# Attention's output stored unnormalised and scaled ahead of the first expert layer, row maxima placed by ScalarE

## The chip, the core and the metric

The kernel runs on one core of a Trainium2 chip. The metric is the device time of one execution in microseconds, as the median of several runs. TensorE (PE) multiplies matrices, VectorE (DVE), ScalarE (ACT) and GpSimd (POOL) work on tiles in SBUF, the first two on PSUM also, and SyncE's queue (SP) issues all DMAs here. The engines run their own instruction lists in order and wait for one another through semaphores.

## What is computed

Attention with rotary positions over 4 batches of 8 heads, 576 positions, 64 columns; its result, brought to 2304 tokens of 512 columns, goes through two expert layers without bias. All is in 32-bit floats.

```python
q_rot, k_rot = rotate(q), rotate(k)
scores = (1 / sqrt(64)) * q_rot @ k_rot.T
attn = exp(scores - max(scores, axis=-1))
attn = attn / (sum(attn, axis=-1) + 1e-9)
x = (attn @ v), heads side by side          # [2304, 512]
h = x @ w_in1;  x = (h - tanh(h)) @ w_out1   # 512 -> 2048 -> 512
h = x @ w_in2;  x = (h * sigmoid(1.702 h)) @ w_out2
```

## The kernel before, in words

**Attention.** 32 heads in 16 pairs. A product of 32-bit accuracy is made of parts: each operand is cut into an upper part (a copy by ScalarE into the format fp32r, `keys_hi` L551, `queries_hi` L557) and a lower part (the rest, a subtraction by VectorE, `keys_lo` L679, `queries_lo` L684). VectorE also rotates keys and queries (`rope`, L659 to L662).

In step h of the loop TensorE computes the transposed scores of head h in five tiles of 128 keys (`scores`, L431 and L437), and with a lag of two tiles the product of the exponentials with v (`probs_v`, L449). Between them it makes scores in the other orientation for the heads ahead (`near_scores`, L414): tiles 1 to 4 of head h+1 in the first two places, tile 0 of head h+2 at the end of the step. VectorE takes the row maxima of these (`row_max`, L667), TensorE transposes the five columns of maxima in the place t = 2 (`maxima_across`, L421), and `place_maxima` (L674, VectorE) multiplies the transposed rows with a 0/1 mask into five rows of `q_max`, where row t holds only the maxima of queries in tile t. The L437 matmuls against the rows of ones in `k_one` then subtract the maxima inside the scores' sum. The slots for scores, near scores and the transpose are three pairs of PSUM banks used in rotation, in the order of `ring_order` (L46 to L60): an operation waits until the third before it in that order has been read.

ScalarE's step h is: exp of each of the five tiles (L537), the copy of the previous head's output `copy_pv` (L545) at t = 1, the cut of x (L580) at t = 2 in the steps 17 and 19, the cut of weights (L573) at t = 3 in the steps 21, 23, 25, 27 and 31, then `keys_hi` at t = 3 and `queries_hi` at t = 4 for head h+3. VectorE's step h is: row maxima 1 to 4 of head h+1, one rope, `place_maxima`, the early cuts, `keys_lo` and `queries_lo` of head h+3, row maximum 0 of head h+2, and in even steps `invert` (L688).

**From attention to x.** v carries 64 columns of ones, so rows of `pv_sb` hold the sums. SP fetches a row of sums per head (`fetch_sums`, L231), VectorE adds 1e-9 and inverts, SP stores the inverses (`store_inverse`, L236), reads them back spread over 64 partitions twice (`spread_inverse`, L244), GpSimd multiplies (`normalise`, L382), and SP stores the pair (`store_x`, L249). `copy_pv` of a head waits until the buffer of four heads before has been multiplied.

**Expert layers.** 2304 tokens in 6 units of 384, 16 steps j per unit. `first_product` (L485) makes h for a step in 12 matmuls, ScalarE the tanh or sigmoid (L608, L610), VectorE g (L742), ScalarE its upper part (L617), VectorE its lower part (L747), `second_product` (L500, L503) another 12 or 9 matmuls, one step behind. At step 8 ScalarE and VectorE cut x for the next unit (L580, L703). In unit 0 they also cut the weights, five steps ahead (L573, L697). x of layer one is read in 768 KB pieces from DRAM by `load_x` (L261), half a unit or more ahead.

Of the kernel before, what the change touches and what calls it, by code (L numbers as in the profile page):

```python
# [6 lines left out]
F32 = mybir.dt.float32  # L7
# [58 lines left out]
def program(nc, q, k, v, w_in1, w_out1, w_in2, w_out2, cos_t, sin_t, out):  # L66
# [3 lines left out]
    inv_scratch = nc.dram_tensor("inv_scratch", [PAIRS, 2, SEQ], F32, kind="Internal").ap()  # L70
# [3 lines left out]
    with ExitStack() as ctx:  # L74
# [41 lines left out]
        inv_wide = [sb(f"inv_wide{j}", [P, SEQ], stack=one_stack) for j in range(2)]  # L116
        x_out = [sb(f"x_out{j}", [P, SEQ], stack=one_stack) for j in range(2)]
# [33 lines left out]
        inv_out = sem("inv_out")  # L151
        inv_in = [sem(f"inv_in{j}") for j in range(2)]
        norm_done = sem("norm_done")
        x_stored = [sem(f"x_stored{j}") for j in range(2)]
# [43 lines left out]
        def _(sp):  # L198
# [26 lines left out]
            def fetch_sums(h):  # L225
# [3 lines left out]
                if pair >= 2:  # L229
                    sp.wait_ge(inv_out, 16 * (pair - 1))  # L230
# [3 lines left out]
            def store_inverse(pair):  # L234
                sp.wait_ge(inv_done, pair + 1)
                sp.dma_start(inv_scratch[pair].rearrange("a (p j) -> (a p) j", j=SEQ // HD), sums[pair % 2][:, :]).then_inc(inv_out, 16)  # L236

            def spread_inverse(pair):
                par = pair % 2
                sp.wait_ge(inv_out, 16 * (pair + 1))  # L240
                if pair >= 2:
                    sp.wait_ge(norm_done, pair - 1)
                for a in range(2):
                    sp.dma_start(inv_wide[par][own(a), :], inv_scratch[pair, a:a + 1, :].broadcast_to([HD, SEQ])).then_inc(inv_in[par], 16)  # L244

            def store_x(pair):
                row, col = pair % PAIRS_PER_BATCH * P, pair // PAIRS_PER_BATCH * SEQ
                sp.wait_ge(norm_done, pair + 1)
                sp.dma_start(x_scratch[0][row:row + P, col:col + SEQ], x_out[pair % 2][:, :]).then_inc(x_stored[pair % 2], 16)  # L249

            def load_x(m, u):
# [3 lines left out]
                if m:  # L255
                    sp.wait_ge(y_stored, 16 * (u + 1))
                else:
                    batches = ((u + 1) * UNIT - 1) // SEQ + 1
                    for j in range(2):
# [24 lines left out]
            for h in range(-1, NHEADS):  # L284
# [27 lines left out]
            store_x(PAIRS - 2)  # L312
# [14 lines left out]
            spread_inverse(PAIRS - 1)  # L327
            for m in range(LAYERS):
                for u in range(UNITS):
# [25 lines left out]
        def _(pool):  # L355
# [5 lines left out]
            nc.gpsimd.memset(tile_mask, 0.0).then_inc(pool_chain, 1)  # L361
            pool.wait_ge(pool_chain, 2)
            nc.gpsimd.affine_select(out=tile_mask, in_=tile_mask, compare_op=ALU.not_equal, fill=1.0,
# [450 lines left out]
```

## Time and profile before

| | us |
|---|---|
| median of 3 runs | 1148.81 (1148.41 to 1148.97) |
| the profiled execution | 1147.27 |
| its span, first to last instruction | 1145.5 |
| mean granted TensorE clock | 0.997 |

Times in a profile count from the start of the span. A line of the timeline gives start, length in us, engine, code line, operation, output<-input and shapes; in square brackets how long the engine stood idle just before, and what released it. "x4" is four instructions told in one line. PEld is TensorE loading weights, which runs beside its matmuls. PEclk is the granted clock, 1.00 for full speed.

### The profile page before, as it was taken

Reading aid. Unit: us, or ns where it says so; the run is one execution under the profiler, and the core shown is the slowest. Engines: PE = TensorE matmul, PEld = TensorE weight load, DVE = VectorE, ACT = ScalarE, POOL = GpSimd, SP = SyncE. Lnnn points to the kernel's source line nnn. Section 1 sums busy time; section 2 is a strip of 40 time slices with the busy share of each in tenths; the row PEclk is TensorE's granted clock in tenths of the full one; section 3 lists DMA queues with packets and bytes.
Section 4 is the critical chain, followed back from the end, with each engine's and each line's share of the span. In section 5 each row is a group of like instructions: output and inputs, shape, how many; then the busy total and the mean of one; then the engine's idle time right before and its main releaser. Section 6 shows DMA issues by size and latency. Waiting matters only on the chain.

```text
span 1145.5 us, 15078 instructions
## 1 busy us (share of the span) xinstructions
PE 1104.1 (96%) x5952; PEld 1017.8 (89%) x5952; DVE 552.4 (48%) x879; ACT 425.7 (37%) x747; POOL 57.1 (5%) x62
## 2 busy tenths in 40 slices
PE   2999998999999999999999999999999999999998
PEld 1888877787789999999999999999999999999997
DVE  7888887888736433232233333455232322323222
ACT  2555554555544423222222323445232222323222
POOL 3011111102111000000000000000000000000000
PEclk9999999999999999999999999999999999999999
DMA  6355557566315300000000100062000000000000
GB/s 182 95 158 127 155 154 201 136 169 166 87 61 178 102 28 29 28 28 11 19 28 28 29 28 28 1 193 83 28 28 28 28 1 28 28 28 1 28 1 28
DMA packets 78854, 79.85 MB, mean 70 GB/s; under 512 B 30144, under 2 KB 55744, under 8 KB 78784
## 3 DMA queue, kind: packets, MB, share of 16 engines
q1 hardware_dynamic: 78784, 78.89, 24.1%
q8 instruction: 47, 0.77, 0.3%
q14 instruction: 23, 0.19, 0.1%
HBM read 55.12 MB, written 14.23 MB: 61 GB/s over the span
## 4 chain that ended last, share of the span: by engine, by line
PE 89%; DVE 7%; SPq 1%; DMA 1%; POOL 1%; issue 1%; ACT 0%; POOLq 0%; DVEq 0%; ACTq 0%
PE PS L485 35%; PE PS L503 17%; PE PS L500 17%; PE PS L449 10%; PE PS L414 3%; PE PS L431 3%; PE PS L437 3%; DVE neg_max L667 2%; DVE q_max L684 1%; DVE k_hl L679 1%; DVE q_max L674 1%; DMA turned_k<-k_dram 1%; DVE raw_q L662 0%; DVE w_parts L697 0%; DVE raw_q L660 0%
## 5 line engine op out<-in xcount | busy, mean ns | idle before, releaser
L485 PE MATMUL PS<-x_hi,w_parts 128*128 128x384 f32 x1536 | 423.1, 336 | 0.0
L742 DVE TENSOR_TENSOR g_raw<-PS,act_t 128x384 f32<-128x384 f32 x192 | 107.0, 557 | 400.2 <-ACT act_t L610 202.1
L485 PEld LDWEIGHTS PS<-x_hi,w_parts 128*128 128x128 f32 x1536 | 280.5, 188 | 4.3
L485 PE MATMUL PS<-x_lo,w_parts 128*128 128x384 f32 x768 | 257.2, 335 | 0.0
L500 PE MATMUL PS<-g_hi,w_parts 128*128 128x384 f32 x768 | 210.3, 334 | 0.8 <-DVE g_lo L747 0.8
L503 PE MATMUL PS<-w_parts,g_hi 128*128 128x512 f32 x576 | 195.1, 393 | 1.0 <-DVE y_sb L756 0.8
L449 PE MATMUL PS<-probs,v_one 128*128 128x288 f32 x640 | 183.4, 409 | 0.3 <-ACT pv_sb L545 0.3
L747 DVE TENSOR_TENSOR g_lo<-g_raw,g_hi 128x384 fp32r<-128x384 f32 x192 | 107.7, 561 | 113.6 <-ACT g_hi L617 113.6
L537 ACT ACTIVATE probs<-PS 128x576 f32<-128x576 f32 x160 | 104.0, 650 | 129.6 <-PE PS L437 126.3
L485 PEld LDWEIGHTS PS<-x_lo,w_parts 128*128 128x128 f32 x768 | 144.2, 188 | 4.2
L617 ACT ACTIVATE g_hi<-g_raw 128x384 fp32r<-128x384 f32 x192 | 100.8, 525 | 122.9 <-DVE g_raw L742 119.7
L500 PEld LDWEIGHTS PS<-g_hi,w_parts 128*128 128x128 f32 x768 | 140.0, 188 | 1.1 <-DVE g_lo L747 1.1
L449 PEld LDWEIGHTS PS<-probs,v_one 128*128 128x128 f32 x640 | 112.4, 191 | 18.1 <-issue 0.5
L667 DVE TENSOR_REDUCE neg_max<-PS 128x1 f32<-128x576 f32 x160 | 113.8, 746 | 30.1 <-PE PS L414 29.5
L500 PE MATMUL PS<-g_lo,w_parts 128*128 128x384 f32 x384 | 128.3, 334 | 0.0
L503 PEld LDWEIGHTS PS<-w_parts,g_hi 128*128 128x128 f32 x576 | 108.1, 188 | 21.9 <-issue 1.1
L610 ACT ACTIVATE act_t<-PS 128x384 f32<-128x384 f32 x96 | 47.2, 492 | 212.5 <-PE PS L485 212.5
L608 ACT ACTIVATE act_t<-PS 128x384 f32<-128x384 f32 x96 | 47.2, 492 | 206.9 <-PE PS L485 206.9
L414 PE MATMUL PS<-k_hl,q_hh 128*128 128x288 f32 x320 | 86.7, 376 | 34.8 <-DMA q_hh<-q_hh 17.5
L503 PE MATMUL PS<-w_parts,g_lo 128*128 128x512 f32 x288 | 113.7, 395 | 0.0
L414 PEld LDWEIGHTS PS<-k_hl,q_hh 128*128 128x128 f32 x320 | 56.4, 200 | 51.8 <-issue 19.7
L431 PE MATMUL PS<-q_hh,k_hl 128*128 128x288 f32 x320 | 80.0, 332 | 0.0
(51 smaller groups left out, 741.3 us busy)
## 6 DMA issues: line engine op xcount, KB each, us to landing
x_raw<-x_scratch SPq DMA_DIRECT2D x12, 768.0 KB, 4.5
raw_w<-moe_w_in_dram SPq DMA_DIRECT2D x32, 256.0 KB, 3.1
raw_w<-moe_w_out_dram SPq DMA_DIRECT2D x32, 256.0 KB, 3.3
raw_k<-k_dram SPq DMA_DIRECT2D x16, 288.0 KB, 3.5
turned_k<-k_dram SPq DMA_DIRECT2D x64, 72.0 KB, 3.2
raw_q<-q_dram SPq DMA_DIRECT2D x16, 288.0 KB, 3.8
turned_q<-q_dram SPq DMA_DIRECT2D x64, 72.0 KB, 3.5
k_one<-k_hl SPq DMA_DIRECT2D x32, 144.0 KB, 2.4
```

The lines of the kernel that those rows point to most:

```text
L414: last = nc.tensor.matmul(slot[:, b, :], q_hh[h % 4][:, t * P:(t + 1) * P], k_hl[h % 4][:, b * HALF:(b + 1) * HALF], start=True, stop=True)
L431: nc.tensor.matmul(slot[:, b, :], k_hl[h % 4][:, keys], q_hh[h % 4][:, b * HALF:(b + 1) * HALF], start=True, stop=False)
L449: last = nc.tensor.matmul(pv_banks[:, b, :], v_one[h // 2 % 2][:, h % 2, t, :], probs[g % PROBS][:, b * HALF:(b + 1) * HALF], start=t == 0 ...
L485: last = nc.tensor.matmul(h_banks[j % 2], w_parts[j][:, w, c * P:(c + 1) * P], x[par][:, c, :], start=(c == 0 and w == 0 and x is x_hi), s ...
L500: last = nc.tensor.matmul(acc_banks[c][:, 0:UNIT], w_parts[j][:, w, c * P:(c + 1) * P], g[:, s, :], start=start, stop=stop)
L503: last = nc.tensor.matmul(acc_banks[c], g[:, s, c * P:(c + 1) * P], w_parts[j][:, w, :], start=start, stop=stop)
L537: nc.scalar.activation(probs[g % PROBS][:, :].rearrange("p (b n) -> p b n", b=2), slot_halves(slot_of("S", h, t)), ACT.Exp).then_inc(exp_d ...
L608: nc.scalar.activation(act_t[:, j % 2, :], h_banks[j % 2], ACT.Tanh).then_inc(act_done, 1)
L617: nc.scalar.activation(g_hi[:, j % STAGES, :], g_raw[:, j % 2, :], ACT.Copy).then_inc(g_hi_done, 1)
L667: nc.vector.tensor_reduce(neg_max[h % 2][:, t:t + 1], slot_halves(slot_of("M", h, t)), AX.XY, ALU.max, negate=True).then_inc(max_done, 1)
L742: nc.vector.tensor_tensor(g_raw[:, j % 2, :], h_banks[j % 2], act_t[:, j % 2, :], ALU.subtract if m == 0 else ALU.mult).then_inc(g_done, 1)
L747: nc.vector.tensor_tensor(g_lo[:, j % STAGES, :], g_raw[:, j % 2, :], g_hi[:, j % STAGES, :].bitcast(F32), ALU.subtract).then_inc(g_lo_don ...
```

## The change

The multiplication by the inverse sums moves. `copy_pv`'s result is stored as it is, per head (`store_x(h)`), GpSimd's `normalise` and SP's `spread_inverse` are gone. The inverses are kept in DRAM by chunk and token; with each `load_x` of the first layer SP loads the inverses spread over 2 x 64 partitions into a new buffer `inverses`, and VectorE multiplies x in place (`scale_x`), early for unit 0 and at step 8 for the others. ScalarE's cut of x waits for it, and its early cut moves from t = 2 to t = 4. `copy_pv` waits for the store of four heads before.

`place_maxima` moves from VectorE to ScalarE: five activations per head of 5x128 with a column of the identity as scale, after the exp of t = 2. The mask and its two GpSimd instructions at the start are gone. The ones in `k_one` cover 576 columns instead of 640.

```diff
@@ sync
-            def spread_inverse(pair):
-                par = pair % 2
-                sp.wait_ge(inv_out, 16 * (pair + 1))
-                if pair >= 2:
-                    sp.wait_ge(norm_done, pair - 1)
-                for a in range(2):
-                    sp.dma_start(inv_wide[par][own(a), :], inv_scratch[pair, a:a + 1, :].broadcast_to([HD, SEQ])).then_inc(inv_in[par], 16)
-
-            def store_x(pair):
-                row, col = pair % PAIRS_PER_BATCH * P, pair // PAIRS_PER_BATCH * SEQ
-                sp.wait_ge(norm_done, pair + 1)
-                sp.dma_start(x_scratch[0][row:row + P, col:col + SEQ], x_out[pair % 2][:, :]).then_inc(x_stored[pair % 2], 16)
+            def store_x(h):
+                pair, a = h // 2, h % 2
+                row, col = pair % PAIRS_PER_BATCH * P + a * HD, pair // PAIRS_PER_BATCH * SEQ
+                sp.wait_ge(pv_copied, h + 1)
+                sp.dma_start(x_scratch[0][row:row + HD, col:col + SEQ], pv_sb[h % 4][own(a), :]).then_inc(x_stored[h % 4], 16)
...
+                if m == 0:
+                    for j in range(2):
+                        sp.wait_ge(inv_out[j], 16 * batches * PAIRS_PER_BATCH // 2)
+                    if u:
+                        sp.wait_ge(x_scaled, u * KC)
+                    for a in range(2):
+                        rows = inv_scratch.rearrange("c a n -> a c n")[a:a + 1, :, u * UNIT:(u + 1) * UNIT]
+                        sp.dma_start(inverses[own(a), :, :], rows.broadcast_to([HD, KC, UNIT])).then_inc(inverses_in, 16)
...
-                if h % 2 and h >= 3:
-                    spread_inverse(h // 2 - 1)
-                if h >= 4 and h % 2 == 0:
-                    store_x(h // 2 - 2)
                 if h >= 1:
                     fetch_sums(h - 1)
+                    store_x(h - 1)
@@ gpsimd
-            nc.gpsimd.memset(tile_mask, 0.0).then_inc(pool_chain, 1)
...
-            def normalise(pair):
...
@@ scalar
             def copy_pv(h):
                 act.wait_ge(pv_done, (h + 1) * TILES)
                 if h >= 4:
-                    act.wait_ge(norm_done, h // 2 - 1)
+                    act.wait_ge(x_stored[h % 4], h // 4 * 16)
...
+            def place_maxima(h):
+
+                act.wait_ge(r_ready, h + 1)
+                for t in range(TILES):
+                    last = nc.scalar.activation(q_max[h % 4][max_rows(h % 2), t * P:(t + 1) * P],
+                                                slot_of("R", h)[0:TILES, 0, 0:P], ACT.Copy, scale=ident[0:TILES, t:t + 1])
+                last.then_inc(row_done, 1)
...
                 for c in chunks:
+                    if m == 0:
+                        act.wait_ge(x_scaled, u * KC + c + 1)
                     nc.scalar.activation(x_hi[par][:, c, :], x_raw[:, c, :], ACT.Copy).then_inc(x_hi_done, 1)
...
-                    if t == 2 and h in early_x:
+                    if t == 2 and 0 <= h + 1 < NHEADS:
+                        place_maxima(h + 1)
+                    if t == 4 and h in early_x:
                         cut_x(0, 0, 0, early_x[h])
@@ vector
-            def place_maxima(h):
...
+            def scale_x(u, chunks=range(KC)):
+                dve.wait_ge(x_loaded, u * 16 + 16)
+                dve.wait_ge(inverses_in, u * 32 + 32)
+                for c in chunks:
+                    nc.vector.tensor_tensor(x_raw[:, c, :], x_raw[:, c, :], inverses[:, c, :], ALU.mult).then_inc(x_scaled, 1)
...
-                if 0 <= h + 1 < NHEADS:
-                    place_maxima(h + 1)
...
                 if h in early_x:
+                    scale_x(0, early_x[h])
                     cut_x(0, 0, 0, early_x[h])
...
                     if j == CUT_AT:
                         if u + 1 < UNITS:
+                            if m == 0:
+                                scale_x(u + 1)
                             cut_x(m, u + 1, 1 - par)
```

## Rows read from the trace of the kernel before

**Rows 1.** The page: engines' busy share, and TensorE's in 40 slices, in tenths

```profile
PE 1104.1 (96%) x5952; PEld 1017.8 (89%) x5952; DVE 552.4 (48%) x879; ACT 425.7 (37%) x747; POOL 57.1 (5%) x62
...
PE   2999998999999999999999999999999999999998
```

**Rows 2.** Busy time by stretch; stretches run from transpose to transpose

```profile
core 0: us, PE busy (x) PEld busy (x) DVE busy (x) ACT busy (x) POOL busy (x), PEclk, DMA share, GB/s
124.70:133.94 9.24, 9.20 (x53) 7.76 (x52) 8.17 (x14) 5.28 (x8) 0.00 (x0) 1.00 0.56 146
133.94:142.90 8.96, 8.96 (x52) 7.75 (x52) 7.83 (x12) 5.16 (x8) 2.81 (x2) 1.00 0.59 151
161.10:172.42 11.32, 9.47 (x52) 7.68 (x52) 10.48 (x14) 5.27 (x8) 3.60 (x2) 1.00 0.36 87
181.41:196.82 15.41, 11.47 (x52) 8.84 (x52) 11.14 (x16) 6.13 (x10) 3.51 (x2) 0.89 0.55 129
215.85:225.92 10.07, 9.21 (x52) 7.77 (x52) 8.90 (x14) 5.87 (x10) 2.83 (x2) 1.00 0.58 152
274.19:284.47 10.28, 9.22 (x52) 7.78 (x52) 9.11 (x13) 5.88 (x9) 2.83 (x2) 1.00 0.73 194
293.72:306.95 13.23, 10.82 (x52) 9.07 (x52) 10.31 (x12) 5.88 (x9) 3.90 (x2) 0.87 0.34 99
193.00:196.00 3.00, 2.87 (x11) 2.35 (x11) 2.78 (x5) 0.70 (x2) 0.00 (x0) 0.54 0.77 152
```

**Rows 3.** Timeline of one ordinary stretch, the step h = 11

```profile
133.94 0.27 PE L421 MATMUL PS<-ident,neg_max 128*5 128x128 f32 x1
...
134.77 0.65 ACT L537 ACTIVATE probs<-PS 128x576 f32<-128x576 f32 x1 [0.96 <-PE PS L437]
...
135.44 0.69 ACT L551 ACTIVATE k_hl<-raw_k 64x576 fp32r<-64x576 f32 x1
...
136.26 0.65 ACT L537 ACTIVATE probs<-PS 128x576 f32<-128x576 f32 x1
...
136.81 0.67 ACT L557 ACTIVATE q_hh<-raw_q 64x576 fp32r<-64x576 f32 x1
...
137.51 0.75 DVE L684 SCALAR_TENSOR_TENSOR q_max<-raw_q,q_hh 64x576 fp32r<-64x576 f32 x1
...
138.19 0.74 DVE L667 TENSOR_REDUCE neg_max<-PS 128x1 f32<-128x576 f32 x1
...
138.58 0.94 PE L414 MATMUL PS<-k_hl,q_hh 128*128 128x288 f32 x4
```

**Rows 4.** Timeline, the same place in the step before (124.70)

```profile
130.03 0.30 PEld L414 LDWEIGHTS PS<-k_hl,q_hh 128*128 128x128 f32 x2 [0.27 <-DVE neg_max L667]
```

**Rows 5.** Timeline, ScalarE's cut of x in a unit of the first layer

```profile
507.46 1.75 ACT L580 ACTIVATE x_hi<-x_raw 128x384 fp32r<-128x384 f32 x4
```

**Rows 6.** Groups of instructions: busy us in all, mean ns, idle before and releaser

```profile
L573 ACT ACTIVATE w_parts<-raw_w 128x1024 fp32r<-128x1024 f32 x32 | 33.5, 1047 | 0.8 <-DMA raw_w<-moe_w_out_dram 0.7
L674 DVE TENSOR_TENSOR q_max<-PS,g_raw 5x640 fp32r<-5x640 f32 x32 | 25.9, 811 | 2.9 <-PE PS L421 2.5
L583 ACT ACTIVATE warm<-ident 128x1 f32<-128x1 f32 x1 | 0.2, 203 | 0.0
```

**Rows 7.** Timeline, VectorE in the disturbed steps h = 14, 16 and 27

```profile
161.53 1.96 DVE L660 TENSOR_TENSOR raw_k<-raw_k,cos_sb 128x576 f32<-128x576 f32 x1
...
191.68 0.17 DVE L691 TENSOR_SCALAR sums<-sums 128x9 f32<-128x9 f32 x1 [2.78 <-DMA sums<-pv_sb]
...
298.08 1.85 DVE L679 TENSOR_TENSOR k_hl<-raw_k,k_hl 64x576 fp32r<-64x576 f32 x1
```

**Rows 8.** Timeline, unit 0 of the first layer at step 8

```profile
376.56 1.96 DVE L703 TENSOR_TENSOR x_lo<-x_raw,x_hi 128x384 fp32r<-128x384 f32 x4
...
380.91 0.33 PE L500 MATMUL PS<-g_hi,w_parts 128*128 128x384 f32 x1
```

**Rows 9.** Timeline of the start

```profile
1.42 0.62 POOL L361 MEMSET g_raw<- 5x640 f32 x1
2.19 0.74 POOL L363 TENSOR_SCALAR_AFFINE_SELECT g_raw<-g_raw 5x640 f32<-5x640 f32 x1
...
17.46 1.78 PE L414 MATMUL PS<-k_hl,q_hh 128*128 128x288 f32 x6 [17.46 <-DMA q_hh<-q_hh]
```

More of the change, by code:

```diff
@@ L96, in program @@
         y_sb = sb("y_sb", [P, KC, BANK])
+        inverses = sb("inverses", [P, KC, UNIT])
         w_parts = [sb(f"w_parts{j}", [P, 4, BANK], F32R) for j in range(APART)]
@@ L150, in program @@
         inv_done = sem("inv_done")
[L151 to L154, printed above, removed]
+        inv_out = [sem(f"inv_out{j}") for j in range(2)]
+        inverses_in = sem("inverses_in")
+        x_scaled = sem("x_scaled")
+        x_stored = [sem(f"x_stored{j}") for j in range(4)]
         raw_w_in = [sem(f"raw_w_in{j}") for j in range(STAGING)]
@@ L229, in fetch_sums @@
                 if pair >= 2:
-                    sp.wait_ge(inv_out, 16 * (pair - 1))
+                    sp.wait_ge(inv_out[pair % 2], 16 * (pair // 2))
                 sp.dma_start(sums[pair % 2][a * HD:(a + 1) * HD, :],
@@ L234, in store_inverse @@
             def store_inverse(pair):
+                row, col = pair % PAIRS_PER_BATCH, pair // PAIRS_PER_BATCH * SEQ
                 sp.wait_ge(inv_done, pair + 1)
-                sp.dma_start(inv_scratch[pair].rearrange("a (p j) -> (a p) j", j=SEQ // HD), sums[pair % 2][:, :]).then_inc(inv_out, 16)
-            def spread_inverse(pair):
-                par = pair % 2
-                sp.wait_ge(inv_out, 16 * (pair + 1))
-                if pair >= 2:
-                    sp.wait_ge(norm_done, pair - 1)
-                for a in range(2):
-                    sp.dma_start(inv_wide[par][own(a), :], inv_scratch[pair, a:a + 1, :].broadcast_to([HD, SEQ])).then_inc(inv_in[par], 16)
-            def store_x(pair):
-                row, col = pair % PAIRS_PER_BATCH * P, pair // PAIRS_PER_BATCH * SEQ
-                sp.wait_ge(norm_done, pair + 1)
-                sp.dma_start(x_scratch[0][row:row + P, col:col + SEQ], x_out[pair % 2][:, :]).then_inc(x_stored[pair % 2], 16)
+                sp.dma_start(inv_scratch[row, :, col:col + SEQ].rearrange("a (p j) -> a p j", p=HD), sums[pair % 2][:, :]).then_inc(inv_out[pair % 2], 16)
+            def store_x(h):
[3 more added lines that the diff above has]
+                sp.dma_start(x_scratch[0][row:row + HD, col:col + SEQ], pv_sb[h % 4][own(a), :]).then_inc(x_stored[h % 4], 16)
             def load_x(m, u):
@@ L258, in load_x @@
                     batches = ((u + 1) * UNIT - 1) // SEQ + 1
-                    for j in range(2):
+                    for j in range(4):
                         sp.wait_ge(x_stored[j], 16 * batches * PAIRS_PER_BATCH // 2)
@@ L373, in _ @@
                 nc.gpsimd.memset(v_one[j][:, :, FULL, :], 0.0).then_inc(cleared, 1)
-            def normalise(pair):
-                par = pair % 2
-                pool.wait_ge(inv_in[par], pair // 2 * 32 + 32)
-                pool.wait_ge(pv_copied, 2 * pair + 2)
-                if pair >= 2:
-                    pool.wait_ge(x_stored[par], pair // 2 * 16)
-                for a in range(2):
-                    last = nc.gpsimd.tensor_tensor(x_out[par][own(a), :], pv_sb[(2 * pair + a) % 4][own(a), :],
-                                                   inv_wide[par][own(a), :], ALU.mult)
-                last.then_inc(norm_done, 1)
-                pool.wait_ge(norm_done, pair + 1)
-            for pair in range(PAIRS - 1):
-                normalise(pair)
-            normalise(PAIRS - 1)
         @block.tensor
@@ L567, in cut_weights @@
                 if m == 0 and c == 13:
-                    act.wait_ge(x_stored[0], 16 * (PAIRS // 2))
-                    act.wait_ge(x_stored[1], 16 * (PAIRS // 2))
+                    for j in range(4):
+                        act.wait_ge(x_stored[j], 16 * (NHEADS // 4))
                 if m:
@@ L707, in _ @@
                 dve.wait_ge(cleared, j + 1)
-                last = nc.vector.memset(k_one[j][max_rows(j % 2), :].bitcast(F32), 1.0)
+                last = nc.vector.memset(k_one[j][max_rows(j % 2), 0:SEQ].bitcast(F32), 1.0)
             last.then_inc(pads_set, 1)
```

17 lines of the change are left out of this document (2 added, 15 removed).

## The prediction, made before the change was timed

> **What bounds the kernel now.** I read the page's busy shares first [rows 1]: TensorE is busy 96% of the span, VectorE 48%, ScalarE 37%. The share hides two stages. In the slices of the span TensorE's row is 9 throughout from the twelfth slice on, and the chain of waits there is nothing but matmuls: the expert layers can only get longer. The row's other digits, 8 to 9, are attention. The stretches in rows 2 cut the attention stage from one head's transpose of maxima (L421) to the next. An undisturbed head takes 9.24 or 8.96 us in turn, with TensorE busy through 9.20 and 8.96 us of it. Eight stretches take longer: 11.32, 15.41, 10.07, 10.28 (this one three times, within 0.02) and 13.23 us are in rows 2, and one of 10.04 (h = 18). (I number a stretch by the loop's step h in which its first transpose stands, which is of head h+1: after it come tiles 3 and 4 of head h and the preparation of h+3. After the two ordinary ones rows 2 have h = 14, 16, 19, 25, 27 and a piece for the clock.) VectorE is busy 8.17 and 7.83 us of an ordinary head, ScalarE 5.2 us. So ScalarE looks idle; the order of its work decides, not its share.
>
> **The chain inside one head.** I then read one head in order of time [rows 3]; R is the transpose's start, 133.94. ScalarE's exp of tile 3 starts at R+0.83, the upper key part (L551) at R+1.50, exp of tile 4 at R+2.32, the upper query part (L557) at R+2.87, ending at R+3.54. VectorE's lower query part (L684) starts 0.03 later, R+3.57, and the first row maximum of head h+2 (L667) after it, R+4.25 to 4.99. TensorE's L414 group at R+4.64 has two tiles; the weights of its second go in at about R+4.99, because the slot is that of the maximum just taken. In the other parity this is an open wait: 0.27 us at R+5.33 [rows 4]. So the chain exp, L551, exp, L557, L684, L667, L414 has no slack left behind L557, and from that L414 on the next transpose follows in a fixed 3.9 to 4.0 us (8.96 less 4.99; 9.24 less 5.33). The only slack is ahead of the second exp: L551 takes 0.69 us of the 0.82 between the two starts, and copies back to back overlap (four of 384 columns in 1.75 us at 0.51 each, so 0.413 apart and 0.10 overlapped [rows 5]). That is 0.13 + 0.10, about 0.22 us.
>
> **The maxima on ScalarE.** Removed: one VectorE operation of 811 ns per head [rows 6], behind rope, 32 times, 25.9 us. It lies where VectorE would otherwise wait for ScalarE's L551 and L557, so taking it away moves nothing in an ordinary head. Added: five ScalarE activations per head of 5x128, in program order ahead of the exp of tile 3. They can start when the transpose has landed: R+0.31 (0.27 long, then 0.04 from an end to its waiter, as at 134.77). No row of before shows an activation of this width or with a scale taken from SBUF. A 1-column activation takes 203 ns [rows 6] and a 576-column one 650 [rows 3], so 128 columns would take 203 + 127 x 0.78 = 302 ns. From below: they overlap as the copies do, one every 0.206 us. From above: they come no faster than the 384-column copies, 0.413. I take 0.30, no gain from overlapping, since each takes another scale column; a scalar fetched per instruction is something the copies don't have. Five of them: 1.5 us (1.03 to 2.07). The exp of tile 3 then starts at R+1.81 instead of 0.83, 0.98 late; less the slack of 0.22, L557 and everything behind it come 0.76 us later (0.29 to 1.33). Behind the waiting ScalarE are queued exp 3, L551, exp 4, L557; for them wait TensorE's slots (tile 3's exp would end at R+2.46, and its slot is wanted at about R+3.2, so that is covered) and VectorE (L684, then L667, then TensorE's L414: not covered). The slot of the transposed row comes free at R+1.9, about a microsecond before the next tile of L414 wants it and earlier than VectorE leaves it now: no loss.
> The Trainium skill (ScalarE: Activation LUTs, "What ACT_TABLE_LOAD costs") says that an activation with immediate operands takes 186 ns + 0.833 ns per column, that each [128,1] pointer operand adds about 93 ns, and that successive ones overlap by about 93 ns. The first and last agree with rows 3 and 5; the pointer is in no row here. By it 128 columns with a pointer scale are 386 ns, one every 0.293, so 0.73 us per head instead of 0.76: nearly the same sum. Without its pointer term the gap would be the 0.20 of the lower bound.
> Ordinary heads: h = 0 to 28 prepare keys and queries. Without h = 14, 16, 17, 19, 21, 23, 25, 27, there are 21: 21 x 0.76 = +16.0 us. One of them, h = 18, already took about 0.8 more than 9.24 and so has that much less to lose: -0.8.
>
> **Heads that also cut weights** (h = 21, 23, 25, 27). ScalarE's cut (1047 ns, less 0.10 of overlap [rows 6]) comes ahead of L551, VectorE's behind it. In the stretch of 10.28 us the first maximum started at about R+5.56 (10.28 less 3.97 and its own 0.75). With exp 3 at R+1.81, VectorE's cut starts at R+3.56, keys, queries follow, and the maximum starts at R+6.2: 0.6 later in three heads, +1.8. The fourth (13.23 us) lost 2.95 more than its like because GpSimd's multiplication stood beside VectorE: a subtraction took 1.85 us [rows 7], where the like of it in rows 3 takes 0.75, and TensorE stood for 2.4 us (13.23 less 10.82 busy [rows 2]). That goes: 10.28 + 0.6 = 10.88, -2.35.
>
> **GpSimd's multiplication gone.** Two per pair, 3.60 us for both in the stretch of h = 14 [rows 2]. Beside them a rope product took 1.96 us [rows 7]; the head falls from 11.32 to 9.24 + 0.76 = 10.0: -1.3. In h = 16 (15.41 us) several things met: SP waited for GpSimd before it issued the next sums, so VectorE's inversion waited 2.78 us for them [rows 7]; the copies of keys and queries were late behind 8 weight loads and 10 others. SP now has no such wait and one DMA fewer per pair (two spreads and one store out, two stores in). I leave 0.7 us for the transfers still crowding there: 10.7, so -4.7. If they crowd as before, only about -3.
>
> **x scaled on VectorE.** Early, in h = 17 and 19: ScalarE's cut of x moves behind exp 4 and waits for VectorE's two products (0.47 apart), which wait for rope; L557 then waits for the cut, VectorE has 2 + 2 extra operations. Followed through, L667 ends at R+7.25 instead of about R+5.0 (h = 17) and R+6.1 (h = 19): +2.2 and +1.2, +3.4 together. TensorE's idle stretch of 2.3 us there is like the one of h = 27, and after those of h = 16 the granted clock of the next 3 us was 0.54, which is 1.2 GHz for most of it [rows 2]; such a drop cost about 1.9 us (matmul groups at about twice their time for some 3.5 us). I charge one: +1.9.
> In the first layer, products of x for units 1 to 5 stand at step 8. In unit 0 of before, VectorE's cut of x ran from 376.56 for 1.96 us and TensorE wanted the step's last product at 380.91 [rows 8]; with 1.88 to 1.96 us of scaling ahead of it the lower part of g ends at 382.0: +1.1, once. In the other units no weights are cut and the same sum ends 0.4 us before TensorE wants it: 0. If that cover were gone it would be 0.5 each. The two loads of inverses per unit stand behind the load of x, half a unit ahead of need: 0. The first pair, at h = 12, moves 0.8 MB more between copies that have over 6 us to land: 0 (up to 2).
>
> **Start.** The mask on GpSimd (0.62 + 0.74 us) leaves the chain to the first L414 at 17.46 [rows 9]; SP, with its loads, gives back only 1.1 of it. In the head before the first, VectorE has 0.81 less on a chain that it bounds, against 0.6 on ScalarE: -1.2 by my count. Together -2.3. Stores per head instead of per pair: heads wait for the store of four heads ago, 36 us earlier: 0.
>
> **The sum.** 16.0 - 0.8 + 1.8 - 2.35 - 1.3 - 4.7 + 3.4 + 1.9 - 2.3 + 1.1 = +12.7 us on a profiled execution of 1147.27 us (span 1145.5, 1.8 around it), 1160.0. That execution is 1.5 us under the median of the runs, 1148.81; on the median it is 1161.5. I say 1161.
>
> **Rivals.** (1) The five activations overlap fully and a scale from SBUF costs nothing: 0.206 apart, 0.29 us per head. 21 heads +6.1, h = 18 -0.8, weights +0.4 and -2.8, h = 14 -1.8, h = 16 -5.2, x +2.5, no clock loss, start -2.5, unit 0 +1.1: -3.0, 1145.8. Faster from about 0.22 apart down. For it: everything else ScalarE does in a row overlaps. Against: nothing shown has a scale operand. This is the side opposite to my forecast. Chance 0.13. (2) In between, 0.22 to 0.26 apart, the per-head loss of 0.36 to 0.56 is balanced by the disturbed heads: 1147 to 1154; chance 0.17. (3) The activations cost more than 0.30, or the repeated wait of 0.7 to 1 us a head brings the clock down in more heads than one (h = 14 stood idle for 1.85 at a clock of 1.00, h = 27 for 2.4 at 0.87 [rows 2]): with 0.34 apart +4 us, each drop +1.9: 1165 to 1175, at 0.413 about 1180; chance 0.20. (4) The disturbed heads stay disturbed, since the transfers and not GpSimd held them: h = 16 and 27 give 3 instead of 7: 1165. It lies in the forecast's spread. The forecast, 1157 to 1165, has 0.50.
>
> **Chances and range.** About 0.2% (2.3 us) is what a measurement of this kernel can tell. Faster, below 1146.5: rival 1 and 0.02 of rival 2, 0.15. Within it: 0.07, out of rival 2. Slower: 0.78, the rest of rival 2, the forecast and rival 3. The range, 1146 to 1172, leaves out half of rival 1 and the upper end of 3.
>
> **What would show it.** Right: in an ordinary head the stretch is 9.6 to 9.9 us, L684 waits for L557, and TensorE's L414 waits for the row maximum 0.5 us or more in every head; the five activations span about 1.5 us. VectorE's operations all have their own length. Wrong: exp of tile 3 by R+1.4; heads of 9.0 to 9.2 us; a longer unit 1 to 5 in the first layer.

## The result, and the profile after

The changed kernel takes 1156.16 us in the median (1153.6 to 1157.57, 4 runs), the kernel before, timed beside it, 1148.66: a ratio of 1.0063 (95% interval 1.0044 to 1.0082), slower by 7.5 us. The forecast was 1161, slower, with a range of 1146 to 1172. The profiled execution took 1153.6, with a span of 1151.8, 6.3 us over that of before. It was the shortest of the four runs. The kernel before varied by 0.6 us in the four runs timed here, and by up to 4.7 us (1145.0 to 1149.7) in those timed beside the later experiments, so one execution tells little of a difference of a few microseconds. The experiments below have the letters a to n; each ratio is to the kernel before as timed beside it.

The page of the changed kernel, to be read against [rows 1]: GpSimd's work is gone, ScalarE has more.

```profile
PE 1103.2 (96%) x5952; PEld 1016.1 (88%) x5952; DVE 531.4 (46%) x871; ACT 464.5 (40%) x907; POOL 7.5 (1%) x28
```

The stretches from one transpose of maxima to the next, as in [rows 2] (columns are the same): two ordinary steps, h = 10 and 11, then h = 14, 16, 19, 25 and 27.

```profile
128.43:138.26 9.83, 9.20 (x53) 7.76 (x52) 7.44 (x13) 6.52 (x13) 0.00 (x0) 1.00 0.54 94
138.26:147.70 9.44, 9.19 (x53) 7.75 (x53) 7.06 (x11) 6.29 (x13) 0.00 (x0) 1.00 0.58 155
166.98:177.76 10.78, 9.18 (x52) 7.65 (x52) 7.83 (x13) 6.51 (x13) 0.00 (x0) 1.00 0.70 157
187.20:197.03 9.83, 9.19 (x53) 7.66 (x53) 7.74 (x13) 6.51 (x13) 0.00 (x0) 1.00 0.71 155
217.99:229.11 11.12, 9.20 (x52) 7.76 (x52) 9.03 (x15) 7.00 (x15) 0.00 (x0) 1.00 0.52 130
280.09:290.83 10.74, 9.19 (x53) 7.75 (x52) 8.29 (x12) 7.12 (x14) 0.00 (x0) 1.00 0.69 187
300.67:311.41 10.74, 9.21 (x53) 7.77 (x52) 8.13 (x11) 7.12 (x14) 0.00 (x0) 1.00 0.35 92
```

Every ordinary step is longer, 9.83 and 9.44 where it was 9.24 and 8.96, and TensorE has idle time in each (9.83 less 9.20 busy). The disturbed steps h = 16 (15.41) and h = 27 (13.23) have become like their neighbours. VectorE is busy 7.4 of 9.8 us, less than before: it is not its load that makes the step longer.

The timeline of the step from 128.43 (h = 10) shows the chain; it answers to [rows 3] (h = 11) and, in the same parity, [rows 4]. L525 are the five activations, L511 exp, L533 and L539 the upper key and query parts, L663 the lower query part, L653 the row maximum, L388 the matmuls of the next heads' scores. R is 128.43.

```profile
128.43 0.27 PE L395 MATMUL PS<-ident,neg_max 128*5 128x128 f32 x1
...
128.74 1.36 ACT L525 ACTIVATE q_max<-PS,ident 5x128 fp32r<-5x128 f32 x5 [0.43 <-PE PS L395]
...
130.00 0.63 ACT L511 ACTIVATE probs<-PS 128x576 f32<-128x576 f32 x1
...
130.66 0.68 ACT L533 ACTIVATE k_hl<-raw_k 64x576 fp32r<-64x576 f32 x1
...
131.36 0.66 ACT L511 ACTIVATE probs<-PS 128x576 f32<-128x576 f32 x1
...
132.04 0.68 ACT L539 ACTIVATE q_hh<-raw_q 64x576 fp32r<-64x576 f32 x1
...
132.76 0.76 DVE L663 SCALAR_TENSOR_TENSOR q_max<-raw_q,q_hh 64x576 fp32r<-64x576 f32 x1 [0.64 <-ACT q_hh L539]
...
133.54 0.76 DVE L653 TENSOR_REDUCE neg_max<-PS 128x1 f32<-128x576 f32 x1
...
134.35 0.53 PE L388 MATMUL PS<-k_hl,q_hh 128*128 128x288 f32 x2 [0.63 <-DVE neg_max L653]
```

The activations start at R+0.31, as forecast, and the exp of tile 3 at R+1.57 instead of R+0.83. ScalarE has no gap from there to the query part; VectorE waits 0.64 us for it, TensorE 0.63 us for VectorE. Compared parity by parity, the upper query part ends at R+4.29 instead of R+3.71 in h = 10 and at R+4.02 instead of R+3.54 in h = 11, 0.58 and 0.48 us later, and the two steps are 0.59 and 0.48 us longer.

### The profile page after: what moved, and what is told of

Read it like the earlier page. It is cut to its first block, busy times and chain, and to the rows that moved or that the text cites. A ratio compares the mean times of both kernels' runs of the same rounds, so it can differ in the third digit from the quotient of the medians.

```text
span 1151.8 us, 15169 instructions
## 1 busy us (share of the span) xinstructions
PE 1103.2 (96%) x5952; PEld 1016.1 (88%) x5952; DVE 531.4 (46%) x871; ACT 464.5 (40%) x907; POOL 7.5 (1%) x28
## 4 chain that ended last, share of the span: by engine, by line
PE 82%; ACT 7%; DVE 6%; issue 3%; SPq 1%; DMA 0%; ACTq 0%
PE PS L459 34%; PE PS L477 17%; PE PS L474 17%; PE PS L423 7%; PE PS L388 3%; ACT probs L511 3%; ACT q_max L525 2%; DVE neg_max L653 2%; DVE q_max L663 2%; PE PS L405 2%; PE PS L411 2%; ACT q_hh L539 1%; SPq L202 1%; ACT w_parts L555 1%; DVE k_hl L658 0%
## 5 line engine op out<-in xcount | busy, mean ns | idle before, releaser
L511 ACT ACTIVATE probs<-PS 128x576 f32<-128x576 f32 x160 | 103.5, 647 | 86.5 <-PE PS L411 84.9
L653 DVE TENSOR_REDUCE neg_max<-PS 128x1 f32<-128x576 f32 x160 | 113.4, 746 | 32.0 <-PE PS L388 31.5
L388 PE MATMUL PS<-k_hl,q_hh 128*128 128x288 f32 x320 | 87.3, 374 | 40.6 <-DVE neg_max L653 21.6
L388 PEld LDWEIGHTS PS<-k_hl,q_hh 128*128 128x128 f32 x320 | 55.8, 197 | 57.9 <-DVE neg_max L653 28.8
```

The costliest lines, as they stand in the source:

```text
L388: last = nc.tensor.matmul(slot[:, b, :], q_hh[h % 4][:, t * P:(t + 1) * P], k_hl[h % 4][:, b * HALF:(b + 1) * HALF], start=True, stop=True)
L511: nc.scalar.activation(probs[g % PROBS][:, :].rearrange("p (b n) -> p b n", b=2), slot_halves(slot_of("S", h, t)), ACT.Exp).then_inc(exp_d ...
L653: nc.vector.tensor_reduce(neg_max[h % 2][:, t:t + 1], slot_halves(slot_of("M", h, t)), AX.XY, ALU.max, negate=True).then_inc(max_done, 1)
```

## The experiments

**The maxima back on VectorE, the rest changed** (a_maxima_on_vector).

```diff
-                    if t == 2 and 0 <= h + 1 < NHEADS:
-                        place_maxima(h + 1)          # ScalarE, five activations
...
+                if 0 <= h + 1 < NHEADS:
+                    place_maxima(h + 1)              # VectorE, behind rope, with tile_mask
```

> The changed kernel, but the maxima are placed by VectorE with the mask, as before. Theory: the whole loss is the five activations ahead of the exp of tile 3, and moving the normalisation is a gain. Then ordinary steps return to 9.24 / 8.96 us (22 x 0.54 = -12), the four weight steps to 10.28 (-2), the start gives back 1.4: about 13 us under the changed kernel, ratio to the kernel before 0.991 to 0.995, with no step of 11.3 or 15.4 us left. Rival: the loss comes from the stores per head, the loads of inverses or the scaling of x; then it stays at 1.003 to 1.006 and ordinary steps are still 9.4 to 9.8.

Measured: 1146.17 us, ratio 0.9981 (0.9971 to 0.999). Stretches of the steps h = 10, 14 and 17:

```profile
126.04:135.30 9.26, 9.23 (x53) 7.79 (x52) 8.16 (x14) 5.26 (x8) 0.00 (x0) 1.00 0.57 100
162.50:175.98 13.48, 10.82 (x53) 8.95 (x53) 8.57 (x14) 5.26 (x8) 0.00 (x0) 0.87 0.66 157
194.20:207.10 12.90, 10.83 (x53) 9.07 (x52) 10.46 (x17) 5.98 (x10) 0.00 (x0) 0.87 0.44 116
```

Ordinary steps are back at 9.26 and 8.97: what made them long is the placing by ScalarE. But the total missed my 0.991 to 0.995. A step of 13.5 us is there that I had said would not be (VectorE's rope waited 2.53 us for a transfer of keys), and h = 17 and 19, with x scaled ahead of the chain, take 12.9 and 11.3. In h = 14 and 17 about 1.6 us of this is the lower granted clock (TensorE is busy 10.8 us instead of 9.2). So the moved normalisation gains little by itself: it takes GpSimd's disturbances away and brings two of its own.

**The placing by ScalarE alone, in the kernel before** (b_maxima_on_scalar): `place_maxima` as in the change, the early cut of x at t = 4, GpSimd's normalisation kept.

```diff
+                    if t == 2 and 0 <= h + 1 < NHEADS:
+                        place_maxima(h + 1)          # ScalarE
-                    if t == 2 and h in early_x:
+                    if t == 4 and h in early_x:
...
-                if 0 <= h + 1 < NHEADS:
-                    place_maxima(h + 1)              # VectorE
```

> The kernel before, but with the maxima placed by ScalarE in five activations. Theory: ordinary steps 9.83 / 9.43 instead of 9.24 / 8.96, 22 x 0.54 = +12, weight steps +0.5 each, start -1.4; the steps disturbed by GpSimd stay or shrink by what the longer period gives: +8 to +13 us, ratio 1.007 to 1.011. Rival (loss from the moved normalisation): ratio 0.998 to 1.000.

Measured: 1164.32 us, ratio 1.0134 (1.0119 to 1.0149), +15.7 us, more than the 8 to 13 I expected. Ordinary steps are 9.82 and 9.45 in turn (the first of them below), as expected. Of the steps disturbed by GpSimd, h = 14 and 16 shrank by 1.0 and 0.8 us, to 10.33 and 14.65; h = 17 and 19, which cut x, grew by 2.3 and 4.8, to 11.26 and 14.88. In h = 19 the multiplication came beside VectorE's lower query part, which now stands last on the chain, and the clock fell to 0.77 of full speed in the stretch:

```profile
129.34:139.16 9.82, 9.20 (x52) 7.76 (x52) 7.45 (x13) 6.50 (x13) 0.00 (x0) 1.00 0.53 136
223.38:238.26 14.88, 11.83 (x52) 10.08 (x52) 9.99 (x14) 6.99 (x15) 3.21 (x2) 0.77 0.40 114
...
228.98 3.27 POOL L377 TENSOR_TENSOR x_out<-pv_sb,inv_wide 64x576 f32<-64x576 f32 x2 [16.47 <-DMA inv_wide<-inv_scratch]
229.10 1.88 DVE L682 SCALAR_TENSOR_TENSOR q_max<-raw_q,q_hh 64x576 fp32r<-64x576 f32 x1
```

The two parts of the change are therefore a loss of about 15.7 us and a gain of 2.5, and together +7.5, 6 us better than their sum. In the profiled executions the difference lies mostly in the steps that cut x: placing on ScalarE adds 7.1 us to h = 17 and 19 where GpSimd multiplies (this kernel against the one before), and takes 1.9 off where VectorE scales x (the changed kernel against a; 1.6 of it is a drop of the clock in a). The cut of x at t = 4 was moved together with the placing here, and no run separates the two.

**Another order on ScalarE** (c_scalar_order).

```diff
+                    if t == 2 and h + PREPARED < NHEADS:
+                        keys_hi(h + PREPARED)
                     if t == 2 and 0 <= h + 1 < NHEADS:
                         place_maxima(h + 1)
+                    if t == 3 and h in early_w:
+                        cut_weights(0, early_w[h])
+                    if t == 3 and h + PREPARED < NHEADS:
+                        queries_hi(h + PREPARED)
                     if t == 4 and h in early_x:
                         cut_x(0, 0, 0, early_x[h])
-                    if t == 3 and h in early_w:
-                        cut_weights(0, early_w[h])
-                    if h + PREPARED < NHEADS:
-                        if t == 3:
-                            keys_hi(h + PREPARED)
-                        if t == 4:
-                            queries_hi(h + PREPARED)
```

> The changed kernel with another order on ScalarE alone: upper key part before the five placing activations, upper query part right behind the exp of tile 3, ahead of the exp of tile 4 (the weight cut stays ahead of the query part). Theory: what hurts is only that the query part comes late for VectorE and its row maximum for TensorE's L388; then the waits of 0.22 and 0.63 us of L388 for the row maximum go in ordinary steps, steps of 8.96 to 9.0, 22 x 0.65 = -14 us against the changed kernel, ratio 0.993 to 0.996. Rival: ScalarE has too much work in that stretch whatever the order (exp late for TensorE's slots): steps stay over 9.3 and L388 or L405 wait for ScalarE's exp.

Measured: 1143.78 us, ratio 0.9956 (0.994 to 0.9973). The stretches h = 10, 11, 17 and 21, and the chain in the first of them:

```profile
130.37:139.31 8.94, 8.94 (x53) 7.73 (x52) 7.12 (x11) 6.41 (x14) 0.00 (x0) 1.00 0.63 161
139.31:148.27 8.96, 8.96 (x53) 7.75 (x53) 7.60 (x13) 6.51 (x14) 0.00 (x0) 1.00 0.55 98
187.09:200.10 13.01, 10.79 (x53) 9.12 (x53) 10.13 (x16) 7.57 (x16) 0.00 (x0) 0.87 0.48 124
231.01:242.06 11.05, 9.20 (x52) 7.68 (x52) 8.30 (x12) 7.23 (x15) 0.00 (x0) 1.00 0.64 178
...
130.99 1.36 ACT L525 ACTIVATE q_max<-PS,ident 5x128 fp32r<-5x128 f32 x5
...
132.92 0.67 ACT L539 ACTIVATE q_hh<-raw_q 64x576 fp32r<-64x576 f32 x1
...
134.29 0.75 DVE L652 TENSOR_REDUCE neg_max<-PS 128x1 f32<-128x576 f32 x1
...
135.02 0.90 PE L388 MATMUL PS<-k_hl,q_hh 128*128 128x288 f32 x4
```

The same work, the same 1.36 us of placing, and TensorE idles nowhere in an ordinary step: 8.94 of 8.94 us. The row maximum starts at R+3.92 instead of R+5.11, 0.33 earlier even than in [rows 3]. So ScalarE's load is no obstacle (6.5 of 8.95 us), only when the query part comes. The five activations still stand ahead of it: what moved is the key part, into the time in which ScalarE had waited for the transpose (it starts 0.10 us before R), and the exp of tile 4, behind the query part. The steps with cuts lost: 13.01 and 13.02 us in h = 17 and 19, 11.05 in h = 21, 23 and 25, 12.65 in h = 27. The cuts still stand ahead of the query part or of VectorE's lower parts, and in h = 17, 19 and 27 about 1.6 us is the lower granted clock (0.87).

**Placing without the scale column** (d_immediate_scale).

```diff
-                                                slot_of("R", h)[0:TILES, 0, 0:P], ACT.Copy, scale=ident[0:TILES, t:t + 1])
+                                                slot_of("R", h)[0:TILES, 0, 0:P], ACT.Copy)
```

> The changed kernel with the five activations as plain copies, without the scale column, so each row of q_max holds the maxima of all tiles (the softmax's shift is not the reference's). Theory: a scale fetched from SBUF is what makes them 345 ns long and 254 apart; plain ones are about 300 and 206 apart, 0.24 us per head, 28 x 0.24 = -7 us against the changed kernel, ratio 0.999 to 1.002. Rival: the scale costs nothing, the length is that of a 5x128 activation; then as the changed kernel, 1.004 to 1.008.

Measured: 1144.6 us, ratio 0.9967 (0.9954 to 0.998). The groups of the five activations, in the changed kernel and in this one:

```profile
L525 ACT ACTIVATE q_max<-PS,ident 5x128 fp32r<-5x128 f32 x160 | 43.5, 345 | 21.9 <-PE PS L395 21.9
```

```profile
L525 ACT ACTIVATE q_max<-PS 5x128 fp32r<-5x128 f32 x160 | 28.7, 253 | 21.0 <-PE PS L395 21.0
...
123.21:132.59 9.38, 9.22 (x53) 7.77 (x53) 7.46 (x13) 6.05 (x13) 0.00 (x0) 1.00 0.56 99
132.59:141.72 9.13, 9.13 (x53) 7.78 (x53) 7.11 (x11) 5.95 (x13) 0.00 (x0) 1.00 0.60 160
```

A scale fetched from SBUF costs 92 ns per activation, 0.46 us per head, and the step falls by as much where it has it to lose (9.83 to 9.38; 9.44 to 9.13). This confirms the elasticity: what ScalarE has ahead of the query part comes out of TensorE's time one to one. The effect was larger than I expected, since a plain 5x128 activation is 253 ns, not 302, and five of them span 0.90 us, one every 0.162 instead of 0.206. The Trainium skill (ScalarE: Activation LUTs, "What ACT_TABLE_LOAD costs") gives 93 ns for such an operand; the traces agree to 1 ns.

**The first loads of x and of the inverses two steps apart** (e_split_loads).

```diff
-                if h == 12:
-                    load_x(0, 0)                     # x, then inverses
+                if h == 10:
+                    load_x(0, 0)
+                if h == 12:
+                    load_inverses(0)
```

> The changed kernel with the first load of x issued at step 10 and the first loads of inverses at step 12, instead of both at step 12. Theory: the 768 KB of x and 768 KB of inverses together are what makes the next loads of keys and queries land in 6.5 us instead of 3.5 and step 14 wait for them; apart, steps 10 to 14 take 9.43 / 9.84 like the others, 1 to 4 us gained (step 14 took 10.78 in the profiled execution and more in slower ones), ratio 1.003 to 1.005, and the times of its runs lie closer together than the 4 us of the changed kernel. Rival: step 14 waits because the queue or the late query part holds the copies back; then nothing changes, 1.005 to 1.007.

Measured: 1154.65 us (four of five runs from 1154.4 to 1154.9, the profiled one 1160.3), ratio 1.0067 (1.0045 to 1.009). Landing times of the transfers issued from 145 us on, first in the kernel before (to 165 us), then in the changed kernel (to 170); the last number is the median from issue to landing. With them stands what VectorE waited for in step h = 14 of the changed kernel:

```profile
turned_k<-k_dram SPq DMA_DIRECT2D x4, 72.0 KB, 5.0
```

```profile
inverses<-inv_scratch SPq DMA_DIRECT2D x2, 384.0 KB, 8.9
...
turned_k<-k_dram SPq DMA_DIRECT2D x4, 72.0 KB, 8.7
...
168.26 0.76 DVE L645 TENSOR_TENSOR turned_k<-turned_k,sin_sb 128x576 f32<-128x576 f32 x1 [1.44 <-DMA turned_k<-k_dram]
```

And the steps h = 14, 16 and 17 of this experiment, with VectorE's wait in h = 16:

```profile
168.58:178.42 9.84, 9.21 (x53) 7.77 (x53) 7.45 (x13) 6.51 (x13) 0.00 (x0) 1.00 0.42 88
187.85:200.51 12.66, 10.79 (x52) 8.96 (x52) 7.84 (x13) 6.51 (x13) 0.00 (x0) 0.87 0.79 181
200.51:213.25 12.74, 10.82 (x52) 9.07 (x52) 9.09 (x15) 7.00 (x15) 0.00 (x0) 0.87 0.31 77
...
190.01 0.76 DVE L651 TENSOR_TENSOR turned_k<-turned_k,sin_sb 128x576 f32<-128x576 f32 x1 [2.31 <-DMA turned_k<-k_dram]
```

The total did not move, as the rival had it. Step 14 was cured (9.84). In the profiled execution step 16 then waited 2.31 us for its keys, which were loaded after the eight weight loads of step 14, and the clock fell in 16, 17 and 19; but that execution was 5.7 us longer than the median, so what kept the other four from gaining is not shown. That the inverses crowd the keys, which my prediction had put at nothing, is shown by step 14 of all profiled executions in which GpSimd is quiet: 10.8 to 13.5 us where both are loaded at h = 12 (the changed kernel, a, c, d and g), 8.94 to 9.84 where they are two steps apart (e, h and k).

**The early cuts behind the chain** (g_cuts_behind): on top of c_scalar_order.

```diff
+        early_scale = {16: (0,), 17: (1,), 18: (2,), 19: (3,)}
-        early_x = {17: (0, 1), 19: (2, 3)}
+        early_x = {17: (0,), 18: (1,), 19: (2,), 20: (3,)}
...
-                    if t == 3 and h in early_w:      # ScalarE
+                    if t == 4 and h in early_w:
...
                 if h % 2 == 0 and h >= 2:
                     invert(h // 2 - 1)
+                if h in early_scale:
+                    scale_x(0, early_scale[h])
+                if h in early_x:                     # moved from ahead of keys_lo
+                    cut_x(0, 0, 0, early_x[h])
+                if h in early_w:
+                    cut_weights(0, early_w[h])
```

> The kernel c_scalar_order, with the early cuts moved off the chain: on ScalarE behind the exp of tile 4, on VectorE behind row maximum 0 and the inversion; x scaled one chunk per step in 16 to 19 and cut one chunk per step in 17 to 20. Theory: the cuts cost c its steps of 13.0 (17, 19), 11.05 (21, 23, 25) and 12.65 (27) because they stand ahead of the lower parts; behind them these steps take 9.0 to 9.5: 8.2 + 6.3 + 3.7 less 4 for the rest = -12 to -16 us, ratio 0.982 to 0.986. Rival: VectorE has no room for them anywhere (8.2 of 8.95 us busy); then the waits only move to the next row maxima and the gain is under 5 us.

Measured: 1129.58 us, ratio 0.9842 (0.982 to 0.9864). Stretches h = 14, 16 and 27:

```profile
157.84:169.59 11.75, 9.18 (x52) 7.64 (x52) 7.84 (x13) 6.48 (x14) 0.00 (x0) 1.00 0.75 164
178.55:188.93 10.38, 9.20 (x53) 7.67 (x53) 8.18 (x14) 6.50 (x14) 0.00 (x0) 1.00 0.81 156
279.45:288.66 9.21, 9.21 (x53) 7.82 (x53) 8.09 (x11) 7.22 (x15) 0.00 (x0) 1.00 0.41 107
```

The cut steps, 13.0, 11.05 and 12.65 in c, are 8.95 to 9.4. With the same busy time on VectorE (8.1 us in h = 27), a weight cut costs TensorE up to 0.25 us instead of 2.1, or 3.7 in c's h = 27 with its drop of the clock. What is left are the waits for transfers in 14 and 16, where VectorE waited 2.31 and 1.60 us for keys.

**Loads spread out and x scaled one step earlier as well** (h_all_moved): on top of g_cuts_behind.

```diff
-                if h == 14:
-                    for c in range(STAGING):
-                        load_w(0, c)
+                if h in (14, 16, 18, 20):
+                    load_w(0, (h - 14) // 2)
...                                                  # and the split loads of e_split_loads
+                    if j == CUT_AT - 1 and m == 0 and u + 1 < UNITS:
+                        scale_x(u + 1)               # one step earlier than the cut
```

> g_cuts_behind with the first load of x at step 10 and its inverses at step 12, the first four weight chunks loaded one per even step from 14 to 20 instead of all at step 14, and x of the next unit scaled at step 7 of each unit instead of 8. Theory: steps 14 and 16 lose their waits for transfers (2 + 1 us), unit 0 its wait of 1.0 us for g: -4 us against g, ratio 0.979 to 0.983. Rival: these waits come back elsewhere; as g.

Measured: 1124.89 us (1123.25 to 1125.64), ratio 0.9797 (0.9779 to 0.9815): the fastest version, 23 us under the kernel before. Steps 14 and 16:

```profile
156.30:165.24 8.94, 8.94 (x53) 7.73 (x53) 7.60 (x13) 6.51 (x14) 0.00 (x0) 1.00 0.49 102
174.19:183.12 8.93, 8.93 (x52) 7.72 (x52) 7.92 (x14) 6.50 (x14) 0.00 (x0) 1.00 0.50 103
```

Here all crowds are spread at once, and both waits go (2.81 and 1.45 us against g), and so does unit 0's wait of 0.98 us for g, which is in g's trace and not in this one. Another 1.5 us between the two profiled executions lies at the start, where the two programs are the same; its cause is open.

**The same with the maxima on VectorE** (k_vector_maxima_moved): h_all_moved with `place_maxima` and the mask as in a_maxima_on_vector.

> h_all_moved but with the maxima placed by VectorE (with the mask), so the placing stands between rope and the lower parts. Theory: with ScalarE's parts early, VectorE's own chain rope, placing, two lower parts, row maximum ends at R+5.0 where TensorE wants it at R+4.99: ordinary steps 9.0 to 9.3, and the steps with cuts over 9.5 since VectorE is busy 8.2 + 1.2 of 9 us; start 1.4 us later; 4 to 10 us slower than h, ratio 0.984 to 0.991. Rival: placing costs the same wherever it stands once ScalarE's order is right: within 1.5 us of h.

Measured: 1128.27 us, ratio 0.9827 (0.9811 to 0.9843), 3.4 us slower than h. The steps of one parity are 9.02 instead of 8.94 (124.52 to 133.54 below), the cut steps 9.2 to 9.6, and the first transpose stands at 23.02, 1.0 later. In the right order the placing on ScalarE is a small gain. In the profiled executions, 5.4 us apart, 3.6 of it is at the start (some of that varies between executions of the same code, see h) and 1.2 in the steps with cuts or scaling. That is less than the 4 to 10 us I gave it.

```profile
124.52:133.54 9.02, 9.02 (x53) 7.76 (x53) 8.17 (x14) 5.27 (x9) 0.00 (x0) 1.00 0.49 94
```

**The kernel before with ScalarE's order alone** (m_before_order): `keys_hi` at t = 2, `queries_hi` behind the exp of tile 3, nothing else.

> The kernel before with ScalarE's order alone changed: upper key part at t = 2, upper query part right behind the exp of tile 3; maxima on VectorE, normalisation on GpSimd. Theory: the chain through the query part is what ordinary steps wait for even there, so steps of 9.24 fall to 9.02 as in k_vector_maxima_moved (14 steps, -3 us); steps with cuts and the ones GpSimd disturbs stay: ratio 0.996 to 0.999. Rival: VectorE's own chain is the bound in it; no change.

Measured: 1145.15 us, ratio 0.9975 (0.9964 to 0.9986). Most steps of 9.24 are 9.01 to 9.08 (h = 6 below; h = 8 and 12 are 9.23 and 9.44), as expected. The disturbed ones stay long: h = 16 takes 16.30, h = 27 11.63.

```profile
87.88:96.89 9.01, 9.01 (x52) 7.78 (x52) 8.17 (x14) 5.29 (x9) 0.00 (x0) 1.00 0.53 119
```

**And with cuts and weight loads moved** (n_before_order_cuts): m_before_order, the cuts as in g_cuts_behind, the weight loads as in h_all_moved. GpSimd still multiplies.

> The kernel before with that order, the early cuts behind the chain as in g_cuts_behind (one chunk of x per step in 17 to 20) and the weight loads spread over steps 14 to 20. Maxima on VectorE, normalisation on GpSimd. If the gain of h_all_moved (-23 us) is owed to order and spreading alone, this comes to 0.982 to 0.986. If the moved normalisation is needed for it, GpSimd's passes (VectorE operations of 1.8 to 2.0 us instead of 0.75, one or two per pair) keep VectorE, busy 8.2 to 9.5 of 9 us, late in the steps with cuts: 0.988 to 0.995.

Measured: 1141.49 us, ratio 0.9942 (0.9925 to 0.9959). Step h = 18, and what made it long:

```profile
201.62:213.25 11.63, 9.64 (x52) 7.76 (x52) 11.25 (x15) 5.81 (x10) 2.96 (x2) 1.00 0.40 94
...
201.34 3.30 POOL L381 TENSOR_TENSOR x_out<-pv_sb,inv_wide 64x576 f32<-64x576 f32 x2 [17.11 <-issue]
201.38 1.98 DVE L657 TENSOR_TENSOR turned_k<-turned_k,sin_sb 128x576 f32<-128x576 f32 x1
...
203.29 1.97 DVE L658 TENSOR_TENSOR raw_k<-raw_k,cos_sb 128x576 f32<-128x576 f32 x1
```

Two rope products of 0.75 us take nearly 2 us each beside GpSimd's pass, and VectorE is busy 11.25 us in a step that could take 8.95. So order and spreading alone are worth 7 of h's 23 us. The moved normalisation on top of them is worth about 13 (k against this kernel, by their ratios; k also loads the first x two steps earlier), and the placing on ScalarE the last 3. With the normalisation moved, no step of h that prepares a head takes over 9.4 us. The Trainium skill (Advanced Engine Details and Errata, "Mode Summary") says that VectorE's second SBUF port is shared with GpSimd, and that GpSimd's instructions and VectorE's two-port ones block each other. It names only those, and no run here shows whether these products, with two inputs each, are among them. The rows show a delay beside GpSimd and its price, 1.2 us for each operation caught.

## Why the prediction was right, step by step

The sign, the mechanism and its place hold: ScalarE's tile-3 exp is late by the placing, the query part after it, and TensorE pays one to one (c undoes it by order alone, d most of it by length alone). Two terms were too large: the sum missed by 6.4 us in the profiled executions, and by 5 in the median, since the profiled execution was the fastest of the four. By terms, in the profiled executions (span +6.3, forecast +12.7):

| term | forecast | measured |
|---|---|---|
| 21 ordinary steps, h = 18 among them | +16.0 - 0.8 | +10.8 |
| weight steps 21, 23, 25 | +1.8 | +1.4 |
| step 27 | -2.35 | -2.5 |
| step 14 | -1.3 | -0.5 |
| step 16 | -4.7 | -5.6 |
| steps 17 and 19 | +3.4 | +3.2 |
| a drop of the clock | +1.9 | 0 |
| start | -2.3 | -1.7 |
| unit 0 of the first layer | +1.1 | +1.0 |

The term that was mis-sized is the first. I took 0.30 us from one activation to the next; it was 0.254 (five in 1.36 us at 345 ns each). Two of my assumptions were wrong and cancelled by luck: the activations do overlap, by 91 ns, and the scale column adds 92. What is left is the plain activation of 128 columns: 253 ns, not the 302 I read off a line between 1 and 576 columns. The step's loss of 0.76 should have been 5 x 0.254 - 0.52 - 0.22 = 0.53; the stretches show 0.59 and 0.48. By the figures of the Trainium skill that the prediction works out (ScalarE: Activation LUTs, "What ACT_TABLE_LOAD costs") the gap would be 0.293, also too high: for the plain activation they give 293 ns, and 253 was measured. With 0.53 in place of 0.76 the sum would be +7.9.

The clock. This is the second term that was too large. I charged a drop of 1.9 us for the idle time of steps 17 and 19; without it and with 0.53 the sum would be +6.0, against the measured +6.3. In the changed kernel TensorE stood 1.92 us in h = 19 and the granted clock stayed at 1.00. In a, c and e steps with 1.9 to 2.2 us of it show 0.87 (a and c in h = 17, e in h = 16), while g idled 2.57 us in h = 14 and kept 1.00. Where it came it cost 1.6 us (10.8 us busy instead of 9.2). The length of the idle time alone does not tell whether the clock falls, so it is a risk to a step, not a term of a sum.

The transfers. "0 (up to 2)" for the first inverses was wrong in its middle: in the profiled execution 0.95 us (10.78 against 9.83 for its like), in a 4.2 (13.48 against 9.26), 1.6 of it by the clock. I had looked at the time that the keys have to land, over 6 us, and not at how long they take when 1.5 MB stand ahead: 8.7 us. Such waits differ between executions, and the median lies 2.6 us above the profiled one. That this difference comes from them is argued, not shown.

Unit 0 went by the sum. The scaling (L683) and the cut (L688) stand one behind the other, the lower part of g ends at 387.06, and TensorE had waited 0.98 us; units 1 to 4 show nothing. It answers to [rows 8].

```profile
381.62 1.96 DVE L683 TENSOR_TENSOR x_raw<-x_raw,inverses 128x384 f32<-128x384 f32 x4
...
383.49 1.95 DVE L688 TENSOR_TENSOR x_lo<-x_raw,x_hi 128x384 fp32r<-128x384 f32 x4
...
386.50 0.56 DVE L731 TENSOR_TENSOR g_lo<-g_raw,g_hi 128x384 fp32r<-128x384 f32 x1 [0.59 <-ACT g_hi L603]
...
387.12 0.44 PE L474 MATMUL PS<-g_hi,w_parts 128*128 128x384 f32 x1 [0.98 <-DVE g_lo L731]
```

Rival 1 fell: the activations do overlap by 91 ns, but the scale costs. Rival 2 is what happened to the activations: it had them 0.22 to 0.26 apart and a loss of 0.36 to 0.56 us per head, and they were 0.254 apart with a loss of 0.53. I had given it 0.17, and its time, 1147 to 1154, is 2 us short of the measured 1156.16, which lies between it and the band of the forecast, 1157 to 1165. Of rival 3 nothing came in the profiled execution. Rival 4 fell too, since steps 16 and 27 gave 8.1 us and not 3; yet transfers do hold step 14 here and in a, c, d and g, and step 16 in c, e and g.

Of the signs I named, the stretch of 9.6 to 9.9 us and the wait of 0.5 us or more hold in one parity only (9.83 and 0.63; the other has 9.44 and 0.25), and the five activations span 1.36 us, not 1.5. None of the signs of being wrong is there. TensorE's row of slices in [rows 1] I read loosely: it has a 2 in its first slice and an 8 in its last, which bears on no term.

## What to carry to other kernels

An engine that is busy half the time can be the bound through the order of its list: find the operation on it that another engine waits for without slack, and put nothing ahead of it that has slack. Work moved to an idle engine costs what it puts in front of that operation, here 5 x 0.254 us less 0.74 us of slack, and nothing in an ordinary step of c, where other work was moved out of the way of that operation. Optional work (cuts of the next stage, its loads) belongs behind the chain and spread out: the same cuts cost 2 to 4 us a step in front (with the drops of the clock) and at most 0.45 behind. Spreading one crowd of transfers freed the step behind it and not the total (e); with all of them spread both steps came free (h).

## What the runs showed of the hardware

An activation with a scale read from SBUF takes 92 ns longer than with none (345 against 253 ns on 5x128 from PSUM), and five in a row overlap by 91 ns. A two-input VectorE operation of 0.75 us takes 1.85 to 1.98 beside a GpSimd multiplication of 64x576. A load of 72 KB issued behind 1.5 MB of others landed in 8.7 us, behind half of that in 5.0; meanwhile the DMA engines were busy throughout and moved 251 GB/s in the changed kernel (columns as in [rows 2]):

```profile
158.00:167.00 9.00, 8.76 (x50) 7.32 (x49) 6.45 (x10) 6.14 (x13) 0.00 (x0) 1.00 1.05 251
```

A wait of about 2 us by TensorE is sometimes followed by a lower granted clock, 0.87 over the step, and sometimes not: 1.87 us idle in e's h = 16 were followed by 0.51 from 194 to 197 us, which is 1.2 GHz for nearly all of it; after 2.57 us in g's h = 14 it stayed at 1.00.
